# Attention inputs in long contiguous rows, the values as 64-column pairs side by side, and thirteen of the value loads issued from ScalarE

## The reference

```
q_d, k_d, v_d = means of 4 neighbouring positions of q, k, v      # 144 positions
out_d     = softmax(scale * q_d @ k_d.T) @ v_d
out_up    = repeat(out_d, 4)
mask      = |pos_q - pos_k| < 4
out_local = softmax(where(mask, scale * q @ k.T, -1e9)) @ v
x = (out_up + out_local), heads side by side                      # 2304 x 512
x = elu(x @ w_in0) @ w_out0
x = (s * relu(x @ w_in1)**2 + b) @ w_out1
```

## Time and profile before

| | us |
|---|---|
| median of 3 runs | 970.12 |
| lowest, highest | 968.46, 970.82 |
| the profiled execution, first to last instruction | 969.6 |
| of it: attention, until TensorE starts the first layer in earnest | 164.8 |
| of it: the two layers | 804.8 |

### The profile page before, as it was taken

The page is one execution under the profiler, slowest core; times in us unless marked ns, Lnnn a source line. Parts: engine busy times, 40 slices in busy tenths (PEclk is TensorE's granted clock), DMA queues, the critical chain, the costliest instruction groups (busy, mean ns, idle before and its releaser), DMA issues.

```text
span 969.6 us, 16132 instructions
## 1 busy us (share of the span) xinstructions
PE 910.8 (94%) x5936; PEld 859.2 (89%) x5936; DVE 405.1 (42%) x780; ACT 416.7 (43%) x1106; POOL 150.1 (15%) x141
## 2 busy tenths in 40 slices
PE   5676677999999999999999999999999999999998
PEld 4565666999999999999999999999999999999996
DVE  7676675432323323323224244344344343343432
ACT  7667576754434434344346632232232222232222
POOL 4444453750000000000016630000000000000000
PEclk8788798999999999999999999999999999999999
DMA  5546553430000000000014400000000000000000
GB/s 129 148 122 155 135 139 101 141 100 1 1 1 1 0 0 0 0 0 1 1 44 130 124 31 1 1 33 1 1 32 0 33 0 0 32 1 1 33 1 33
DMA packets 71185, 41.42 MB, mean 43 GB/s; under 512 B 41696, under 2 KB 62688, under 8 KB 71136
## 3 DMA queue, kind: packets, MB, share of 16 engines
q1 hardware_dynamic: 71136, 40.78, 15.1%
HBM read 36.05 MB, written 4.72 MB: 42 GB/s over the span
## 4 chain that ended last, share of the span: by engine, by line
PE 84%; SPq 11%; issue 2%; DMA 2%; DVE 1%; ACT 0%; ACTq 0%; DVEq 0%
PE ps_h L503 41%; PE ps_y L524 21%; PE ps_y L522 21%; SPq L256 3%; SPq L240 3%; SPq L250 2%; SPq L251 1%; DMA kpad<-in_kt 1%; DMA wstage<-in_w_in 1%; SPq L242 1%; PE ps_s L411 0%; SPq L252 0%; SPq L255 0%; PE ps_x L455 0%; SPq L262 0%
## 5 line engine op out<-in xcount | busy, mean ns | idle before, releaser
L644 ACT ACTIVATE g_hi<-tmp 128x384 fp32r<-128x384 f32 x192 | 101.0, 526 | 261.9 <-PE ps_y L524 152.2
L503 PE MATMUL ps_h<-xs_hi,win_late_lo 128*128 128x384 f32 x576 | 193.8, 336 | 0.0
L503 PE MATMUL ps_h<-xs_hi,win_late_hi 128*128 128x384 f32 x576 | 193.8, 336 | 0.0
L503 PE MATMUL ps_h<-xs_lo,win_late_hi 128*128 128x384 f32 x576 | 193.6, 336 | 0.0
L793 DVE TENSOR_TENSOR g_lo<-tmp,g_hi 128x384 fp32r<-128x384 f32 x192 | 107.4, 559 | 204.7 <-ACT g_hi L644 204.7
L638 ACT ACTIVATE tmp<-ps_h 128x384 f32<-128x384 f32 x192 | 94.3, 491 | 227.7 <-PE ps_h L503 225.3
L785 DVE SCALAR_TENSOR_TENSOR tmp<-tmp,ps_h 128x384 f32<-128x384 f32 x96 | 53.2, 554 | 161.8 <-ACT tmp L641 161.0
L503 PEld LDWEIGHTS ps_h<-xs_lo,win_late_hi 128*128 128x128 f32 x576 | 108.3, 188 | 3.3
L503 PEld LDWEIGHTS ps_h<-xs_hi,win_late_hi 128*128 128x128 f32 x576 | 108.2, 188 | 3.2
L503 PEld LDWEIGHTS ps_h<-xs_hi,win_late_lo 128*128 128x128 f32 x576 | 108.3, 188 | 0.0
L789 DVE TENSOR_TENSOR tmp<-tmp 128x384 f32<-128x384 f32 x96 | 55.2, 575 | 121.9 <-ACT tmp L638 121.9
(11 more groups left out here) (94 smaller groups left out, 1469.2 us busy)
## 6 DMA issues: line engine op xcount, KB each, us to landing
wstage<-in_w_in SPq DMA_DIRECT2D x32, 256.0 KB, 2.8
wstage<-in_w_out SPq DMA_DIRECT2D x32, 256.0 KB, 2.8
qbd<-in_qt SPq DMA_DIRECT2D x32, 144.0 KB, 3.6
kpad<-in_kt SPq DMA_DIRECT2D x16, 288.0 KB, 3.8
v<-in_v SPq DMA_DIRECT2D x16, 288.0 KB
out<-wstage SPq DMA_DIRECT2D x18, 256.0 KB, 2.2
vwin<-in_v SPq DMA_DIRECT2D x32, 112.0 KB
vwin<-in_v SPq DMA_DIRECT2D x32, 33.5 KB
```

Source lines behind the costliest of these rows:

```text
L503: mm = pe.matmul(o, w_chunk(0, a, j)[:, c * P:(c + 1) * P], xs[x][:, slot, c, :], start=(c == 0 and p == 0), stop=(c == CH - 1 and p == 2))
L644: act.activation(g[0][:, j % 2, :], x, ACT.Copy).then_inc(hi_ready, 1)
```

## The change

- Queries: `qbd` is laid out head by head, so a row of 576 numbers is one run of 2304 bytes instead of nine of 256.
- Keys: `kall` has no zero columns. The windows are clipped to the sequence: the first window begins at position 0 and the last ends at 575 (`WSTART`), so every window has 70 true keys. The mask is adapted: three ranges of tiles for each half, twelve selects instead of four.
- Values: the host places the two heads side by side, so a run is 512 bytes for `vwin` and 2048 for `v4`. The transfers of a pair are still seven (`NV`): 64 and 6 partitions for the seven inner tiles, the same for each of the two edge tiles, and the one of `v4`.
- `vwin`, `vd`, `probt` and `probdt` have 70 or 72 partitions, so nothing beneath is cleared, and the zero fills and waits for them are gone.
- The values of the pairs 0 to 2 are still loaded by SyncE, ahead of its loop. Those of the pairs 3 to 15 are issued by ScalarE, behind its second copy (L598 before) and ahead of the band exponentials.
- The number of bytes, matmuls, exponentials and vector operations is the same.

The core of the diff:

```diff
-            qbd = sba("qbd", [P, CH, NT, 2, QT])
-            kpad = sba("kpad", [P, CH, KPAD])
-            vwin = sba("vwin", [P, CH, 2, NT, D])
-            v4 = sba("v4", [KD, CH, 2, 2, POOL * D])
+            qbd = sba("qbd", [P, CH, 2, S])
+            kall = sba("kall", [P, CH, S])
+            vwin = sba("vwin", [WIN, CH, NT, 2, D])
+            v4 = sba("v4", [KD, CH, 2, POOL, 2 * D])
...
+        def load_v(eng, bb, slot):
+            vp = v[bb, slot]
+            inner = vp[QT - REACH:QT - REACH + (NT - 2) * QT].rearrange("(t r) x -> r t x", r=QT)
+            rest = vp[2 * QT - REACH:2 * QT - REACH + (NT - 2) * QT].rearrange("(t r) x -> r t x", r=QT)
+            dst = vwin[:, slot].rearrange("p t h d -> p t (h d)")
+            eng.dma_start(dst[0:QT, 1:NT - 1, :], inner).then_inc(v_loaded[slot], 16)
+            eng.dma_start(dst[QT:WIN, 1:NT - 1, :], rest[0:2 * REACH]).then_inc(v_loaded[slot], 16)
+            for t in (0, NT - 1):
+                a = WSTART[t]
+                eng.dma_start(dst[0:QT, t, :], vp[a:a + QT]).then_inc(v_loaded[slot], 16)
+                eng.dma_start(dst[QT:WIN, t, :], vp[a + QT:a + WIN]).then_inc(v_loaded[slot], 16)
+            eng.dma_start(v4[:, slot].rearrange("p k i x -> p k (i x)"),
+                         vp.rearrange("(k p i) x -> p k (i x)", k=2, i=POOL)
+                         ).then_inc(v_loaded[slot], 16)
...
-                if left >= 3:
-                    sp.wait_ge(values_ready, i + 1)
-                    load_v(n + (u + 3) // CH, (u + 3) % CH)
             pairs(sp, step)
...
             for h in range(2):
-                half = band[h * QT:(h + 1) * QT]
-                then(pool.affine_select(out=half, in_=half, compare_op=ALU.is_ge, fill=MASKED, base=0,
-                                        pattern=[[0, NT], [1, WIN]], channel_multiplier=-1))
...
+                for a, z in ((0, 1), (1, NT - 1), (NT - 1, NT)):
+                    low = a * QT - WSTART[a] - REACH
+                    part = band[h * QT:(h + 1) * QT, a:z, :]
+                    then(pool.affine_select(out=part, in_=part, compare_op=ALU.is_ge, fill=MASKED, base=-low,
+                                            pattern=[[0, z - a], [1, WIN]], channel_multiplier=-1))
...
+            last.then_inc(consts_ready, 1)
+            pool.wait_ge(consts_ready, 2)
...
                 act.wait_ge(turned, 4 * i + 2)
                 act.activation(probt[0:WIN, 4:8, :].rearrange("p t x -> p (t x)"), ps_t[0:WIN, 1, :], ACT.Copy).then_inc(turn_copied, 1)
+                if left >= 3:
+                    load_v(act, n + (u + 3) // CH, (u + 3) % CH)
                 if left >= 1:
                     exp_band(n1, u1, last_tiles)
```

More of the change, by code:

```diff
@@ L38, in attention_moe_moe2 @@
     WIN = QT + 2 * REACH
-    KPAD = S + 2 * REACH
     NTA = 5
+    WSTART = [min(max(t * QT - REACH, 0), S - WIN) for t in range(NT)]
     NTX = 5
@@ L55, in attention_moe_moe2 @@
     assert TOK % TB == 0 and DM == 512 and PAIRS == J and PAIRS % 4 == 0
+    NV = 7
     G_CREDIT = 2
@@ L239, in load_qk @@
                     rows = slice(h * D, (h + 1) * D)
-                    sp.dma_start(qbd[rows, slot, :, h, :],
-                                 q_t[bb, 2 * slot + h].rearrange("d (t x) -> d t x", t=NT)).then_inc(qk_loaded[slot], 16)
-                sp.dma_start(kpad[:, slot, REACH:REACH + S],
+                    sp.dma_start(qbd[rows, slot, h, :], q_t[bb, 2 * slot + h]).then_inc(qk_loaded[slot], 16)
+                sp.dma_start(kall[:, slot, :],
                              k_t[bb, 2 * slot:2 * slot + 2].rearrange("h d s -> (h d) s")).then_inc(qk_loaded[slot], 16)
[L245 to L256, removed]
             def load_w(layer, j, half, slot):
@@ L341, in _ @@
             for h in range(2):
-                half = band[h * QT:(h + 1) * QT]
-                then(pool.affine_select(out=half, in_=half, compare_op=ALU.is_ge, fill=MASKED, base=0,
-                                        pattern=[[0, NT], [1, WIN]], channel_multiplier=-1))
[L345 to L348, removed]
+                for a, z in ((0, 1), (1, NT - 1), (NT - 1, NT)):
[3 more added lines that the diff above has]
+                                            pattern=[[0, z - a], [1, WIN]], channel_multiplier=-1))
+                    last = pool.affine_select(out=part, in_=part, compare_op=ALU.is_ge, fill=MASKED, base=low + 2 * REACH,
+                                              pattern=[[0, z - a], [-1, WIN]], channel_multiplier=1)
+                    if h == 0 or z < NT:
+                        then(last)
+            last.then_inc(consts_ready, 1)
+            pool.wait_ge(consts_ready, 2)
             def pool_q(n, u):
                 pool.wait_ge(qk_loaded[u], 48 * (n + 1))
-                x = qbd[:, u].rearrange("p t h (a i) -> p (t h a) i", i=POOL)
+                x = qbd[:, u].rearrange("p h (a i) -> p (h a) i", i=POOL)
                 pool.tensor_tensor(q_half[:, u % 2], x[:, :, 0:2], x[:, :, 2:4], ALU.add).then_inc(q_part, 1)
@@ L410, in scores @@
                     for h in range(2):
-                        mm = pe.matmul(ps_s[h * QT:(h + 1) * QT, bank, a:a + WIN], qbd[:, u, t, h, :],
-                                       kpad[:, u, t * QT:t * QT + WIN], start=True, stop=True)
+                        mm = pe.matmul(ps_s[h * QT:(h + 1) * QT, bank, a:a + WIN], qbd[:, u, h, t * QT:(t + 1) * QT],
+                                       kall[:, u, WSTART[t]:WSTART[t] + WIN], start=True, stop=True)
                 mm.then_inc(scores_ready, 1)
@@ L816 @@
         "in_kt": np.ascontiguousarray(k.transpose(0, 1, 3, 2)),
-        "in_v": np.ascontiguousarray(v),
+        "in_v": np.ascontiguousarray(v.reshape(v.shape[0], v.shape[1] // 2, 2, *v.shape[2:]).transpose(0, 1, 3, 2, 4)).reshape(
+            v.shape[0], v.shape[1] // 2, v.shape[2], 2 * v.shape[3]),
         "in_w_in0": np.ascontiguousarray(moe_w_in),
```

56 lines of the change are left out of this document (21 added, 35 removed).

## The result

Over four runs the changed kernel takes 998.13 us in the median (996.67 to 998.40), the kernel before 969.78 in the same session: a ratio of 1.0292 [1.0277, 1.0308]. The prediction was 962.0 us, faster, with a range to 980. The sign was missed, and the time lies outside the range. The profiled execution spans 996.3 us, 26.7 more than before. The kernel before was timed again in each of the later sessions, with medians from 968.46 to 969.57 us; ratios to "before" are to the median of the same session, and where two versions from different sessions are compared, some 1.3 us can be the session's.

A forecast was written before the change was run, and what follows sets the result against it. SyncE's queue was taken to bound the attention, with ScalarE next. A later start of 0.9 us, 98.2 us of free steps and 13 × 2.8 us of issuing, less 143.6, gave −8.1 us: 962.0 us, range 946 to 980.

The forecast's parts named there:

- The bound of before: In the attention, SyncE's queue sets the 9.14 us step, with a stall at the second 67-partition transfer (2.39 us).
- What goes: SyncE's stall, the scores' waits for keys and 21.3 us of weight-piece waits vanish; SyncE needs about 2.2 us a step.
- the change does not free the loads: Rival: another queue or DMA engine still sets about 9.5 us a step, time stays at 970 us; chance 0.07.
- The gross gain of 45.4 us: ScalarE's 15 attention steps with loads free take 98.2 us instead of 143.6, at 6.6 us for most steps.
- The issues' price: Seven DMA issues on ScalarE take 3.75 us a step, with 0.50 us for each of four edge pieces.
- The cover: ScalarE's two copies, already handed to the datapath, hide 0.97 us of the issuing in each step.
- D: Net time that issuing adds to each of 13 ScalarE steps: 2.8 us, bounds 1.5 to 4.5, break-even 3.42.
- free step: A ScalarE step in which no transfer is late: 6.6 us, ending with a 0.23 us wait for TensorE.
- main case: Issuing on ScalarE adds 2.2 to 3.2 us a step, changing the time by −15.9 to −2.9 us; chance 0.50.
- The rival of the clock: Issues leave TensorE idle, half clock returns 0.5 us a step, 6.5 us in all, 968.5 us; chance 0.05.
- The rival of two queues: SyncE's and ScalarE's issues delay each other, adding 1.7 us a step, 984 us, slower; chance 0.20.
- The start: GpSimd's longer mask, ending at 8.6 us, delays ScalarE's first copy by 0.9 us, bounds 0 and 2.3.

The follow-up runs named there:

- split67: The kernel before with only its two 67-partition value transfers each cut into 64 and 3 partitions; 951.79 us, 0.9820 of before.
- floor: The changed kernel without value loads in the loop, slots filled once and 12 pairs using stale values; 947.17 us in one run.
- layout_sp: The changed kernel with all value loads issued by SyncE again and none by ScalarE; 944.53 us, 0.9740 of before.
- late: The changed kernel with ScalarE's seven issues moved to the end of its step, behind five exponentials; 960.93 us, 0.9918 of before.
- warm13: The changed kernel with 13 extra identity products a step on TensorE, where it waits for ScalarE's last copy; 969.24 us, 1.0024 of before.
- queue_only: The kernel before, old layout kept, with only the value loads of pairs 3 to 15 moved to ScalarE; 1034.74 us, 1.0689 of before.
- half: The changed kernel with the four edge pieces issued by SyncE and three of the seven issues left on ScalarE; 952.62 us, 0.9845 of before.

## Why the prediction was wrong, step by step

- **The bound of before.** Right. SyncE's queue held the steps, and its 67-partition transfers held the queue: split67 shows 16.7 us for them alone.
- **What goes.** Right. No stall, no wait for keys after the first, none for weights; SyncE off the chain, ScalarE's queue on it. The rival "the change does not free the loads" fell.
- **The gross gain of 45.4 us.** Mis-sized. Steps without late loads are 7.7 to 7.8 us (floor, layout_sp), not 6.6; the gain to be had was 24 us. I took 6.6 from two steps in a run in which loads held most of the others, and did not ask what VectorE needs in a step when no step waits; GpSimd's instructions beside it lengthen its own. For the kernel as changed this error did nothing, since ScalarE had become slower than VectorE. It means that the change could not have won much even with cheap issues.
- **The issues' price.** 4.14 us against 3.75: L244 and L245 follow one another at 0.65 and 0.46 to 0.70 us, where I took 0.50. Small.
- **The cover.** The mechanism was right, the size not: 79.81 − 79.10 = 0.71 us after the first copy the issues begin, and the first exponential is 3.93 us later than without them (4.12 in the mean of 13 steps); I had 2.8.
- **D as a whole.** The sum priced D without what follows on TensorE. This is the step that failed. The table adds up, for each kernel, what ScalarE's timeline shows in the mean of its 13 steps with loads, and compares it with the measured step. "Added" is the time from the first copy to the first exponential less the 0.97 us of before; "idle" is the idle time ahead of the next first copy less the 0.23 us of the free step (the wait for transposes, in late the issues themselves).

| kernel | 6.6 + added + idle | sum, us | measured, us |
|---|---|---|---|
| changed kernel | 6.6 + 4.12 + 1.06 | 11.8 | 11.90 |
| warm13 | 6.6 + 3.48 − 0.23 | 9.9 | 9.71 |
| late | 6.6 + 0.02 + 2.45 | 9.1 | 9.07 |
| queue_only | 6.6 + 6.92 + 0.97 | 14.5 | 14.90 |

  So 6.6 + D is the right form wherever ScalarE sets the pace, to within 0.4 us. Held at 2.4 GHz the D of this change is 9.71 − 6.6 = 3.1 us, within my main case (2.2 to 3.2). TensorE's clock adds 2.2: 1.3 as the wait for transposes ahead of the first copy (1.29 in the mean, none in warm13), 0.6 because a sequencer that stands at that wait can't issue ahead (5.09 − 4.45); these rows do not place the last 0.3.
- **The rival of the clock.** I named it, with 0.5 us a step and a chance of 0.05. It was the decisive one and is worth more than four times that. I priced one product group run at half clock. In fact it closes a ring: late issues, late last copy, TensorE idle for 3.9 us, slow pooled scores and transposes, late first copy, later issues. The sign that I named for it, scores at 2.4 us, did not come: the band scores stayed at 258 ns (before 250). The slow ones are those right behind the idle time.
- **The rival of two queues.** It fell. L245 took 0.55 us beside SyncE's query load and 0.37 without, at 83.17; some 0.2 us a step, not 1.7, and half, which has both issuers, takes 0.2 us a step more than layout_sp. It came nearest to the time only by its sign.
- **The start.** 18.81 − 16.40 = 2.4 us against 0.9, beyond my upper bound of 2.3. The mask ended where I put it:

```profile
8.13 0.24 POOL L343 TENSOR_SCALAR_AFFINE_SELECT band<-band 64x70 f32<-64x70 f32 x1
```

  It ends at 8.37 (forecast 8.6), and GpSimd's first use behind it began at 8.46, before at 6.23. The cover that I took off isn't there.
- **The sum.** Forecast for the last copy: −8.1 us; measured 185.90 − 159.96 = +25.9. The difference of 34.0 is 1.5 of the start and 13 × 2.5 = 32.5 of the steps (2.2 for the clock, 0.3 for longer and less covered issues). The last two steps are as forecast, and the layers add 0.8.
- **The rule on several issuers.** By the Trainium skill's rule that the prediction weighed ("DMA: Bandwidth & Descriptors", section "Issuing engines are not separate DMA queues") the move gives nothing, and layout_sp, floor and half bear that out. Its "usually small" does not hold: issuing cost ScalarE some 4.1 us in each step.

## What to carry to other kernels

A DMA issue on a computing engine is work on that engine, in order, and is to be put where the engine's next result is wanted latest: the same seven issues cost 54 us behind a copy that others wait for (against none on SyncE), 16 us at the step's end, and 8 us in the median when only three of them were there (of which the steps explain 3). Before a stalled queue is unloaded onto another engine, look for the one transfer that stalls it; here cutting 67 partitions into 64 and 3 gave 17 us by itself. And ask of each new wait how long it leaves TensorE idle and what it runs next, because the products behind the idle time are on somebody's path.

## What the hardware showed that I had not expected

- A gap of some 4 us on TensorE in each step of 12 held the mean granted clock at 0.73 of 2.4 GHz (pooled scores 465 ns, transposes 392). Thirteen added products a step in that gap held it at 1.00 (294 and 276 ns) and took 29 us off the kernel; twenty-four took off 2 us, which is not clear of noise, as they were in the way.
- GpSimd and VectorE are not independent: one normalisation on VectorE took 1.58 us beside additions on GpSimd and 0.82 without, and one GpSimd instruction less a step took 7 us off (944.5 to 937.5) and some 0.7 us off VectorE's instructions in each step.
- Issues took 0.32 to 0.64 us each in the median, by kind, on ScalarE's sequencer, about as on SyncE's (0.32 to 0.64), and a few kilobytes cost nearly as much as a large one: 0.37 us for 6 partitions of 512 bytes, 0.32 for the 288 KB of `v4`.
